# Fewer weight splits ahead of the slot loop, and two steps moved, in the front part of an attention and expert kernel

## The reference

```python
for t in range(S):
    kt, vt, rt = (k[:, :, t], v[:, :, t], r[:, :, t])
    cur = np.einsum('bhd,bhe->bhde', u[None] * kt, vt)
    y[:, :, t] = np.einsum('bhd,bhde->bhe', rt, state + cur)
    state = w[None, :, :, None] * state + np.einsum('bhd,bhe->bhde', kt, vt)
```

```python
h = x @ w_in                      # 384 -> 2048
x = (h / (1 + np.exp(-h))) @ w_out   # 2048 -> 384
logits = x @ w_gate + modality_bias[modality_id]
e_idx = np.argmax(logits, axis=1)
# for each expert e and its tokens:
out[mask] = gate_w[mask, None] * (np.maximum(x[mask] @ w1[e], 0) @ w2[e])
```

## Time and profile before

| | |
|---|---|
| median of 3 executions | 806.04 us |
| profiled execution's own time | 806.23 us |
| its span, first to last instruction | 804.6 us |
| TensorE matmul busy | 748.8 us (93%) |
| VectorE busy | 511.1 us (64%) |
| ScalarE busy | 436.1 us (54%) |
| GpSimd busy | 226.5 us (28%) |
| mean granted TensorE clock | 0.989 |

### The profile page before, as it was taken

How to read it: one execution, slowest core, us unless ns; L and a number is a source line. 1 busy time by engine, 2 the same in 40 slices (tenths; PEclk the granted TensorE clock), 3 DMA queues, 4 the chain that set the end, 5 groups by cost and what they waited for, 6 DMA issues and landing times. The chain is left out here.

```text
span 804.6 us, 24931 instructions
## 1 busy us (share of the span) xinstructions
PE 748.8 (93%) x9894; PEld 726.4 (90%) x9894; DVE 511.1 (64%) x1349; ACT 436.1 (54%) x1087; POOL 226.5 (28%) x337
## 2 busy tenths in 40 slices
PE   3699999999999999999999999997999999999993
PEld 3588899999999999999999998996899999999992
DVE  7889766766577657855585666216865665566561
ACT  4676454554564546454645455435565555565561
POOL 4532122332214221522151112102423223233321
PEclk9999999999999999999999999998999999999997
DMA  8941222222221222222212210313587656655661
GB/s 317 382 162 50 82 73 94 74 94 75 67 90 49 94 75 94 74 94 74 93 50 82 75 57 3 117 81 118 193 200 252 217 205 226 234 196 201 231 203 69
DMA packets 24159, 104.94 MB, mean 130 GB/s; under 512 B 4411, under 2 KB 9800, under 8 KB 20482
## 3 DMA queue, kind: packets, MB, share of 16 engines
q1 hardware_dynamic: 19362, 93.34, 33.6%
q0 software_dynamic: 4704, 10.29, 4.2%
HBM read 93.90 MB, written 10.11 MB: 129 GB/s over the span
## 5 line engine op out<-in xcount | busy, mean ns | idle before, releaser
L630 ACT ACTIVATE g<-ps_h 128x256 f32<-128x256 f32 x192 | 73.6, 383 | 199.0 <-PE ps_h L1021 145.4
L1019 PE MATMUL ps_h<-x_hi,wi_hi 128*128 128x256 f32 x576 | 165.2, 287 | 5.2 <-DVE x_lo L802 5.2
L1021 PE MATMUL ps_h<-x_hi,wi_lo 128*128 128x256 f32 x576 | 162.9, 283 | 0.9 <-issue 0.9
L1020 PE MATMUL ps_h<-x_lo,wi_hi 128*128 128x256 f32 x576 | 163.0, 283 | 0.0
L1036 PE MATMUL ps_o<-wo_hi,g_hi 128*128 128x392 f32 x384 | 135.4, 353 | 3.5 <-DVE g_lo L835 3.0
L1037 PE MATMUL ps_o<-wo_lo,g_hi 128*128 128x392 f32 x384 | 130.8, 341 | 0.1
L1038 PE MATMUL ps_o<-wo_hi,g_lo 128*128 128x392 f32 x384 | 130.4, 340 | 0.0
L835 DVE TENSOR_TENSOR g_lo<-g,g_hi 128x256 fp32r<-128x256 f32 x192 | 84.8, 446 | 68.9 <-ACT g_hi L623 66.9
L1019 PEld LDWEIGHTS ps_h<-x_hi,wi_hi 128*128 128x128 f32 x576 | 109.1, 189 | 7.7 <-DVE x_lo L802 5.4
L505 POOL TENSOR_TENSOR store<-store,up_half 128x256 f32<-128x256 f32 x44 | 34.5, 784 | 278.9 <-PE ps_y L1006 277.3
L1021 PEld LDWEIGHTS ps_h<-x_hi,wi_lo 128*128 128x128 f32 x576 | 109.2, 190 | 1.1 <-issue 1.1
(11 more groups left out here) (202 smaller groups left out, 1546.5 us busy)
## 6 DMA issues: line engine op xcount, KB each, us to landing
store<-in_w SPq DMA_DIRECT2D x28, 1536.0 KB, 8.9
store<-in_quads SPq DMA_DIRECT2D x48, 704.0 KB, 4.7
x_rows<-rows SPq DMA_DIRECT2D x12, 384.0 KB, 3.2
woT_raw<-in_woT SPq DMA_DIRECT2D x4, 768.0 KB, 10.4
wi_raw<-in_wi SPq DMA_DIRECT2D x4, 768.0 KB, 10.5
wo_raw<-in_wo SPq DMA_DIRECT2D x4, 768.0 KB, 12.3
store<-x_rows,entries POOLq DMA_INDIRECT x26
out_rows<-y,entries_out POOLq DMA_INDIRECT x26
```

Source lines behind the costliest of these rows:

```text
L630: S.activation(g[:, F % 2, :], ps_h[F % 2][:, 0:ETOK], ACT.Silu).then_inc(g_made, 1)
L1019: T.matmul(out, hi, x_hi[:, t % 2, c, :], start=(c == 0), stop=False)
L1020: T.matmul(out, hi, x_lo[:, t % 2, c, :], start=False, stop=False)
L1021: last = T.matmul(out, lo, x_hi[:, t % 2, c, :], start=False, stop=(c == KC - 1))
```

## The change

Two things. The up weights are split four slots ahead in place of six: splits 4 and 5 leave the place ahead of the loop, and inside the loop slot F makes split F + 4, up to slot 11, in place of F + 6, up to slot 9, on ScalarE and on VectorE. And two steps move: on ScalarE `first_states()` goes from ahead of the loop into slot 0, behind `g_high(0)` and ahead of `set_diagonal(4)`; on VectorE `scale(4)` and `sum_bonus(4)` go ahead of `x_low(3)`.

```diff
@@ ScalarE
             x_high(3)
-            first_states()
             wi_high(3)
-            wi_high(4)
-            wi_high(5)
             for F in range(SLOTS):
...
                 silu(F)
                 g_high(F)
+                if F == 0:
+                    first_states()
                 if F in DIAGONAL_AT:
                     set_diagonal(DIAGONAL_AT[F])
-                if F < FCH - 6:
-                    wi_high(F + 6)
+                if F < FCH - 4:
+                    wi_high(F + 4)
@@ VectorE
             wi_low(2)
-            x_low(3)
             scale(4)
             sum_bonus(4)
+            x_low(3)
             wi_low(3)
-            wi_low(4)
-            wi_low(5)
             for F in range(SLOTS):
...
-                if F < FCH - 6:
-                    wi_low(F + 6)
+                if F < FCH - 4:
+                    wi_low(F + 4)
```

## The result

The changed kernel takes 811.65 us (median of 6 executions, 809.21 to 813.39) against 806.13 us for the kernel before (median of 6): ratio 1.0066, 95% interval 1.0046 to 1.0087. It is slower, by about 5.5 us. The profiled execution takes 811.17 us, its span is 809.6 us, 5.0 us more than before.

The account below looks back on a forecast made before the run. VectorE's queue, fed by ScalarE, was taken as the bound through the first token tile, TensorE after it. 3.1 + 0.88 + 0.47 = 4.45 us gave 810.5 us, own range 808.1 to 811.9 us, whole range 807.0 to 812.6 us.

Parts of the forecast that it names:

- Step A: First up product: scale(4) and sum_bonus(4) ahead of x_low(3) delay it 1.55 us, bounds 0.54 and 2.56 us.
- step C: Slots 1 to 5: VectorE's order and collisions with GpSimd stay, 3.1 us passed on, gate_low(1) at 51.9 us.
- plain sum: First up product: the 1.55 us that scale(4) and sum_bonus(4) took before, simply added ahead of x_low(3).
- upper bound's reason: Ahead of first up product: sum_bonus(4) releases GpSimd's next product, now ahead of x_low(3); delay up to 2.56 us.
- Step B: Slot 0: first_states delays ScalarE's queue 2.38 us; VectorE enters its busy stretch 3.1 us late.
- d + 1.5 us: Slot 0: total delay, d from the first up product, plus 2.38 us copies less 0.85 us slack; 2.1 to 4.1 us.
- what would show it: Signs in slot 0: wi_low(4) after 5 us or more idle, set_diagonal(5) released by the bonus near 44.6 us.
- Step D: Slots 10 and 11: the two later up splits cost 0.88 and 0.47 us; bounds nothing to 1.76 us.
- only the first delay counts: Rival: first_states and late splits vanish in idle time; 0.5 to 1.55 us, 806.6 to 807.6 us; chance 0.15.
- larger: Rival: first up product's delay at its upper bound, slots 2 to 4 run slow; 7.3 us, 813.4 us; chance 0.08.
- faster: Rival: TensorE's waits at gate products and flush go, if gate_low(1) is by about 49.4 us; 804.0 us; chance 0.07.

Follow-up runs that it names:

- states alone: Kernel before with only first_states() moved into slot 0, behind g_high(0): ratio 1.0011 (1.0001 to 1.0021).
- states and splits: Changed kernel without its first part: x_low(3) again ahead of scale(4), first_states() in slot 0, splits four slots ahead: ratio to before 1.0034 (1.0022 to 1.0045).
- changed with GpSimd's wait: Changed kernel, but GpSimd waits for x_low(3) before its work on quad 5: ratio to before 1.0038 (1.0025 to 1.0051).
- front-loaded: Kernel before with more up-weight splits in the idle times of slots 0 and 1, then ten slots ahead: ratio 0.9971 (0.9961 to 0.9981).
- states at the end: Kernel before with first_states() in slot 0 behind wo_high(1), at the end of ScalarE's slot: ratio 0.9995 (0.9984 to 1.0005).
- scale first: Kernel before with only scale(4) and sum_bonus(4) moved ahead of x_low(3), the change's first part alone: ratio 1.0040 (1.0027 to 1.0053).
- before with GpSimd's wait: Kernel before, but GpSimd waits for x_low(3) before its work on quad 5: ratio 1.0001 (0.9992 to 1.0009).

## Why the prediction was right

The forecast was 810.5 us, +4.45 us; measured is 811.65 us, +5.5 us (+3.7 to +7.0 by the interval), inside the forecast's own range but only 0.25 us under its end of 811.9 us. The mechanism stands in each step. Two terms were too small, both for the same reason: how VectorE and GpSimd meet was taken as unchanged. Step A is 0.70 us and step C 0.40 us more than forecast, the others together 0.1 us less; that is the 5.4 us of the rows copy.

Step A, forecast 1.55 us with bounds of 0.54 and 2.56 us, is 2.25 us. The plain sum took GpSimd's cost as unchanged. It is not: in the old order GpSimd delayed the three pieces of `x_low(3)` by 1.01 us; in the new one it meets the five operations of `scale(4)` (1.40 us more with the bonus), and then `x_low(3)` as well (1.68 us in place of 1.29). The upper bound's reason was half right: `sum_bonus(4)` no longer was what GpSimd waited for (its load was, until 34.72 us), yet its product then fell beside `x_low(3)`. With GpSimd held back in both orders the delay is 1.43 us: the plain sum prices the order rightly, and what it lacks is GpSimd's part. The Trainium skill (SBUF — State Buffer, "SBUF: two separate sides") gives VectorE and GpSimd one port pair under an exclusive lock. The prediction read from that rule a delay near its upper bound of 2.56 us; the measured 2.25 us lies nearer to that than to the plain sum.

Step B, d + 1.5 us: with the measured d = 2.25 us it gives 3.75 us; `set_diagonal(5)` came 3.70 us late, released by the bonus, and `wi_low(4)` followed an idle time of VectorE of 5.45 us, both as written under what would show it. That the copies hide is refuted by the timeline of the run with them alone; the run with them at the end of the slot shows that it is the queue behind them that pays.

Step C passed on 4.10 us, where 3.7 us came in. The prediction let the collisions stay, since GpSimd would come 2.8 us later and VectorE 3.1 us. GpSimd came 3.31 us later and VectorE's split 3.71 us; so GpSimd's block, which before started together with `wo_low(2)`, now starts 0.41 us ahead of it, and `wo_low(2)` takes 1.09 us in place of 0.55 us. Other runs show the same: where `wo_low(2)` takes 1.09 or 1.10 us (states alone, states and splits, changed with GpSimd's wait, front-loaded, states at the end), it is 6.24 to 6.28 us from the first split of slot 1 to `gate_low(1)`; where it takes 0.55 us and `g_low(1)` 0.97 us (before, scale first, before with GpSimd's wait), 5.85 or 5.86 us.

Step D, 0.88 and 0.47 us, measured 0.88 us (4.97 less 4.09) and 0.44 us (5.41 less 4.97). The run without the first part, 11.56 us in place of 12.38 us, shows that the 0.88 us is not fixed: it hangs on how many operations fall beside GpSimd.

Of the rivals, "only the first delay counts" would have given 0.5 to 1.55 us; the first part alone gave 2.2 to 4.2 us, and the two parts that this rival prices at nothing gave 1.8 to 3.6 us by themselves. The slow stretches of the "larger" rival do occur: in the changed kernel the matmuls of slots 1 and 2 ran at the slower level up to 44.4 us, in the kernel before only up to 39.6 us. No cost is seen there: VectorE ended the scaled keys of quad 5 at 44.87 us, and their scores started at 44.92 us. The prediction read a granted clock of 1.00 around the slow scores; the last section shows why that column can't be relied on there. The "faster" rival wanted `gate_low(1)` at 49.4 us or sooner; it was at 52.91 us, so its condition did not arise.

## What to carry to other kernels

When hand-ordered queues feed each other, price a moved step by what stands behind it in its own queue up to the next time that engine waits for nothing but itself; the same copies delayed `gate_low(1)` by 1.7 us or by 0.6 us within one slot. Price, too, what a moved step will run beside: two engines that slow each other meet differently after every shift, here for 0.4 to 0.8 us a time. Work done ahead in idle time is worth more than its place suggests as long as the engine that does it is the bound later on: two splits fewer ahead cost 0.24%, splits ten slots ahead in place of six gained 0.29%. And an earlier start of the busiest engine gains nothing while another engine's queue is the bound.

## What the runs showed of the hardware

VectorE's subtractions and products with two SBUF inputs take about twice their time beside GpSimd's products, and a delay or gain elsewhere moves the two against each other: 0.42 or 0.82 us for the same `g_low`. GpSimd's fills and counts (MEMSET and IOTA, 28.3 to 30.1 us) have no such cost: three pieces of `x_low` take 1.29 us beside them, and a split that starts beside the last of them at 29.73 us takes 0.56 us in the kernel where GpSimd is then held back, against 1.30 us in the changed kernel, where GpSimd's product follows at 30.03 us.

TensorE fell to the 1.2 GHz level after waits of 1.3 to 2.3 us in six of the thirteen profiles and not in others with the same waits (the changed kernel's 2.06 us, for one). In all six the granted clock is 0.50 or 0.51 in that stretch, and the matmuls of 256 columns start 0.21 us apart in place of 0.12 us. What decides between the two is not known from these runs. At the start of the slot loop the column and the matmuls can differ: the matmuls have the slower spacing in every profile, the granted clock of the stretch is 0.50 with the states alone (33.3 to 42.0 us), and 1.00 in the kernel before (33.4 to 39.8 us). There the durations have to be read, not the column. A slow stretch cost about 1.5 us where TensorE was the bound (scale first); in slot 5 of the run without the first part, where VectorE was, none is seen: 12.17 us from the first to the second `gate_low`, against 12.37 us in the changed kernel.
